# A fused attention and feed-forward kernel: two small loads on ScalarE's queue, one table zeroed by VectorE, and the first w3 tile ahead of w_out

## What is computed

```python
# attention, B=2, H=8, S=768, D=64, 16 centroids for each head
mask = argmax(q_n @ c_n) == argmax(k_n @ c_n)         # both normalised, as the centroids
attn = softmax(where(mask, q @ k.T / sqrt(D), -1e9))
x = (attn @ v)                                        # 1536 tokens x 512
# first feed-forward, d_ff=1024
h = ((x @ w1) * (x @ w2)) @ w3                        # w3: 1024 x 1024
y = h @ w_out                                         # w_out: 1024 x 512
# second feed-forward, d_ff=2048
g = x @ w_in; g = max(g, 0) + alpha * min(g, 0); out = g @ w_out2
```

## Time and profile before

| | us |
|---|---|
| median of three runs | 748.8 |
| the profiled execution | 748.81 |
| its span, first to last instruction | 747.0 |
| TensorE products busy (PE) | 740.9 (99%) |
| TensorE weight loads busy (PEld) | 641.8 (86%) |
| VectorE busy (DVE) | 414.1 (55%) |
| ScalarE busy (ACT) | 312.8 (42%) |
| GpSimd busy (POOL) | 179.7 (24%) |

### The profile page before, as it was taken

One profiled execution on the slowest core, in us unless ns is written; L12 is line 12 of the kernel. 1 busy time (PEld: TensorE's weight loads), 2 busy tenths in 40 slices (PEclk: granted clock), 3 DMA queues, 4 the chain that ended last, 5 costly groups with the idle time before them and its releaser, 6 DMA issues.

```text
span 747.0 us, 10658 instructions
## 1 busy us (share of the span) xinstructions
PE 740.9 (99%) x3792; PEld 641.8 (86%) x3792; DVE 414.1 (55%) x632; ACT 312.8 (42%) x623; POOL 179.7 (24%) x211
## 2 busy tenths in 40 slices
PE   8999999999999999999999999999999999999998
PEld 7888999999999998888888888888888888888886
DVE  4435999999999993721311432475433334343432
ACT  5235988988988884411311332432012111121111
POOL 2141466866865894500000000000000000000000
PEclk9999999999999999999999999999999999999999
DMA  9645476776576332300000032230001000010001
GB/s 296 193 127 126 84 164 135 146 163 150 130 165 152 73 87 84 106 29 1 1 0 1 13 100 70 72 117 25 1 0 57 1 0 1 1 56 1 1 0 57
DMA packets 64859, 55.74 MB, mean 75 GB/s; under 512 B 31520, under 2 KB 53040, under 8 KB 64816
## 3 DMA queue, kind: packets, MB, share of 16 engines
q1 hardware_dynamic: 64816, 55.16, 28.7%
HBM read 31.50 MB, written 3.19 MB: 46 GB/s over the span
## 4 chain that ended last, share of the span: by engine, by line
PE 97%; DVE 1%; POOL 1%; ACT 1%; issue 0%; POOLq 0%; DVEq 0%
PE slot L622 62%; PE acc L622 24%; PE slot L686 9%; PE acc L635 1%; PE slot L734 1%; DVE xl L1160 0%; DVE xl L1142 0%; POOL cwin L465 0%; ACT xh L935 0%; ACT xh L942 0%; POOL oh L466 0%; DVE abx L1280 0%; DVE ab L1276 0%; ACT abx L1052 0%; ACT asb L1038 0%
## 5 line engine op out<-in xcount | busy, mean ns | idle before, releaser
L622 PE MATMUL slot<-xh,w 128*128 128x512 f32 x768 | 247.9, 389 | 0.0
L622 PEld LDWEIGHTS slot<-xh,w 128*128 128x128 f32 x768 | 144.2, 188 | 29.8
L622 PE MATMUL slot<-xl,w 128*128 128x512 f32 x384 | 149.4, 389 | 0.0
L1098 ACT CAST gh<-gf 128x512 fp32r<-128x512 f32 x48 | 29.9, 623 | 203.2 <-PE acc L622 186.0
L1203 DVE TENSOR_TENSOR pl<-slot,ph 128x384 fp32r<-128x384 f32 x192 | 97.5, 549 | 8.4 <-ACT ph L970 8.2
L1197 DVE TENSOR_REDUCE nm<-slot 128x1 f32<-128x768 f32 x96 | 91.1, 949 | 15.3 <-PE slot L622 14.2
L970 ACT CAST ph<-slot 128x384 fp32r<-128x384 f32 x192 | 83.8, 489 | 33.3 <-PE slot L686 32.4
L962 ACT ACTIVATE pf<-slot,nm 128x768 f32<-128x768 f32 x96 | 88.2, 919 | 6.0 <-DVE nm L1197 5.7
L622 PEld LDWEIGHTS slot<-xl,w 128*128 128x128 f32 x384 | 72.1, 188 | 14.9
L1326 DVE TENSOR_TENSOR gl<-gf,gh 128x512 fp32r<-128x512 f32 x48 | 33.2, 692 | 89.9 <-ACT gh L1098 89.9
L622 PE MATMUL slot<-k,q 96*128 96x384 f32 (+1 forms) x384 | 83.0, 337 | 0.0
(11 more groups left out here) (121 smaller groups left out, 1015.9 us busy)
## 6 DMA issues: line engine op xcount, KB each, us to landing
stage<-in_moe_w SPq DMA_DIRECT2D x16, 256.0 KB, 3.2
stage<-in_moe_w_in SPq DMA_DIRECT2D x16, 256.0 KB, 2.7
stage<-in_moe_w_out SPq DMA_DIRECT2D x16, 256.0 KB, 3.0
stage<-in_moe_w SPq DMA_DIRECT2D x6, 512.0 KB, 4.2
qk<-in_q SPq DMA_DIRECT2D x16, 192.0 KB, 4.1
qk<-in_k SPq DMA_DIRECT2D x16, 192.0 KB, 4.3
vn<-in_v SPq DMA_DIRECT2D x16, 192.0 KB, 3.7
q<-k SPq DMA_DIRECT2D x16, 192.0 KB, 2.8
```

The source lines that it names most:

```text
L622: return nc.tensor.matmul(o, a, b, start=start, stop=stop)
L1098: copy(gh[j % 2][:, :], gf[j % 2][:, :]).then_inc(gh_done, 1)
```

## The change

The centroids' and alpha's loads are issued by ScalarE, ahead of its first wait, and no longer by SP. The zeros in `cwin[0]`, which the idle products read, are written by VectorE with a semaphore of their own, `zeroed`, and no longer by GpSimd, whose setup count falls by one. TensorE does 12 and 8 idle products in place of 8 and 6, and waits for the identity after the first group. ScalarE and VectorE take w3 tile 0 ahead of w_out piece 0. In `product_first` the pair with w3's low part comes before the pair with w_out's low part. Everything else is unchanged.

```diff
--- before.py
+++ after.py
@@ -205,7 +205,7 @@
         masked = [sem(f"masked{j}") for j in range(HB)]
         inverted, inverse_out, inverse_in = sem("inverted"), sem("inverse_out"), sem("inverse_in")
         low_in, join_in = ([sem(f"{name}{e}") for e in range(2)] for name in ("low_in", "join_in"))
-        setup_pool, setup_act = sem("setup_pool"), sem("setup_act")
+        setup_pool, setup_act, zeroed = sem("setup_pool"), sem("setup_act"), sem("zeroed")
         cen_turned, table_done = sem("cen_turned"), sem("table_done")
         piece_hi, piece_lo = sem("piece_hi"), sem("piece_lo")
         front_hi, front_lo = sem("front_hi"), sem("front_lo")
@@ -230,7 +230,7 @@
 
         block = ctx.enter_context(nc.Block())
 
-        POOL_SETUP = 16 + HB
+        POOL_SETUP = 15 + HB
         CEN_DVE = 6
         CLUS = 9
         W12_EARLY = len(W12_STEPS)
@@ -239,7 +239,7 @@
         NWO = NF // 2
         READY_W12, READY_W34 = NWO - W12_EARLY, NWO - W12_EARLY + NF
         W3_STAGED = 3
-        IDENT, ZEROS, OPERANDS = 2, 3, 5
+        IDENT, OPERANDS = 2, 4
 
         def staged(e, piece):
 
@@ -379,10 +379,8 @@
                 if c % T6 == 4 and (not last or c // T6 + 2 < HB):
                     next_v(it, c // T6 + 2)
 
-            sp.dma_start(cn[:, :], cen.rearrange("h c d -> (h c) d")).then_inc(ld_cen, 16)
             load_w3(0, 0)
             load_wo(0)
-            sp.dma_start(al16, alpha.rearrange("(j p) -> j p", p=P)).then_inc(ld_al, 16)
             for i in range(1, NWO):
                 load_wo(i)
             load_w3(1, 1)
@@ -454,7 +452,6 @@
             ordered(nc.gpsimd.memset(ident[:, :], 0.0))
             ordered(nc.gpsimd.affine_select(out=ident[:, :], in_=ident[:, :], compare_op=ALU.not_equal, fill=1.0,
                                             base=0, pattern=[[-1, P]], channel_multiplier=1))
-            ordered(nc.gpsimd.memset(cwin[0][:, :].bitcast(F32), 0.0))
             ordered(nc.gpsimd.memset(scl[:, :], 1.0))
             ordered(nc.gpsimd.memset(scl[0:D, :], SCALE))
             ordered(nc.gpsimd.memset(zero[:, :], 0.0))
@@ -751,12 +748,12 @@
                 pe.wait_ge(w3_hi, 1)
                 for g in range(2):
                     mm(o, w3h[:, 0, g, :], woh[:, g, :], g == 0, False)
+                pe.wait_ge(w3_lo, 1)
+                for g in range(2):
+                    mm(o, w3l[:, 0, g, :], woh[:, g, :], False, False)
                 pe.wait_ge(piece_lo, 1)
                 for g in range(2):
                     mm(o, w3h[:, 0, g, :], wol[:, g, :], False, False)
-                pe.wait_ge(w3_lo, 1)
-                for g in range(2):
-                    mm(o, w3l[:, 0, g, :], woh[:, g, :], False, False)
 
             def product_tile(f, parity):
                 pe.wait_ge(w3_lo, f + 1)
@@ -768,14 +765,15 @@
                 for _ in range(n):
                     mm(slot[2][:, 1, 0:HS], cwin[0][:, 0:P], cwin[0][:, 0:HS], True, True)
 
-            pe.wait_ge(setup_pool, ZEROS)
-            spin(8)
+            pe.wait_ge(zeroed, 1)
+            spin(12)
+            pe.wait_ge(setup_pool, IDENT)
             turn_w3(0, 0)
             pe.wait_ge(setup_act, 1)
             nc.tensor.transpose(acc[0:D, 0, 0:P], cn[:, :], ident[:, :])
             pe.wait_ge(ld_al, 16)
             nc.tensor.transpose(acc[:, 1, 0:NJ], al16, ident[0:NJ, 0:NJ]).then_inc(cen_turned, 1)
-            spin(6)
+            spin(8)
             product_first()
             pe.wait_ge(piece_lo, 2)
             product_wc(0, (2, 3))
@@ -922,6 +920,8 @@
         def _(act):
             copy = nc.scalar.copy
 
+            act.dma_start(cn[:, :], cen.rearrange("h c d -> (h c) d")).then_inc(ld_cen, 16)
+            act.dma_start(al16, alpha.rearrange("(j p) -> j p", p=P)).then_inc(ld_al, 16)
             act.wait_ge(ld_cen, 16)
             nc.scalar.activation(xf[0][:, 0, 0:D], cn[:, :], ACT.Square, accum_out=cs[:, 0:1]).then_inc(act_step, 1)
             act.wait_ge(dve_step, 1)
@@ -992,8 +992,8 @@
                     probabilities(it, c)
 
             act.wait_ge(setup_pool, OPERANDS)
+            w3_hi_part(0, 0)
             wo_hi(0)
-            w3_hi_part(0, 0)
             wo_hi(1)
             wo_hi(2)
             wo_hi(3)
@@ -1127,6 +1127,7 @@
                 dve.wait_ge(dve_step, count[0])
 
 
+            nc.vector.memset(f32(cwin[0][:, :]), 0.0).then_inc(zeroed, 1)
             dve.wait_ge(act_step, 1)
             ordered(nc.vector.tensor_scalar_max(cs[:, 1:2], cs[:, 0:1], 2.0 ** -100))
             dve.wait_ge(act_step, 2)
@@ -1226,8 +1227,8 @@
                     inverse(it, j)
 
             dve.wait_ge(setup_pool, OPERANDS)
+            w3_lo_part(0, 0)
             wo_lo(0)
-            w3_lo_part(0, 0)
             wo_lo(1)
             wo_lo(2)
             wo_lo(3)
```

## The result

The changed kernel takes 750.32 us (median of 15 runs, 750.12 to 750.50); the kernel before takes 748.80 in the same comparison. The ratio is 1.0019, with a 95% interval of 1.0013 to 1.0026: 1.5 us slower, a small loss that is clear of the measurement. The profiled execution took 750.23, its span is 748.4 (before: 748.81 and 747.0). The range given was 748.6 to 750.3, so the median lies 0.02 above its upper end, and it is 0.7 above the forecast of 749.6.

What follows compares the result with a forecast made beforehand. TensorE was taken to hold 97% of the chain, so only the start before 11.01 us could move; VectorE's first split 0.81 later gave 748.81 + 0.81 = 749.6 us, range 748.6 to 750.3.

Steps and rivals of the forecast that it cites:

- What bounds the kernel, and that the shift at 11.01 us carries over to the end: TensorE's products of chunk (2, 3) start at 11.01; the rest follows at the same distance, the later chain being TensorE.
- The loads, SP's side: SP's queue: w3 tile issued at 0.73 instead of 1.18, landing about 4.13; early[0] at about 5.8, later ones gain 0.9.
- The table load behind the issues: ScalarE's start: two issues until 1.63, table load of 1.28, Square at 2.92 in place of 2.48.
- The third rival: ScalarE: table load ahead of the two issues, up to +3.3, 752.1; with the second rival 0.14 to 750.3, 0.08 beyond.
- When the centroids land: Centroids on ScalarE's queue: landing bounded at 2.43 to 5.03; up to 3.8 was taken, costing nothing.
- The second rival: ScalarE's Square: centroids queue behind large transfers, landing L shifts L - 3.02; with the third 0.14 to 750.3, 0.08 beyond.
- The zeroed table: VectorE's memset begins at 0.73 and takes 0.35 to 0.42; TensorE's idle products start at about 1.18.
- Twelve idle products, and the clock: TensorE: twelve take 4.00, end at 5.18; transpositions take 1.91 at the lower clock, tile turned at 7.09.
- The first rival: TensorE's clock rises earlier, tile turned as early as 6.21: 748.5 to 749.3, chance 0.26.
- The order on ScalarE and VectorE: Turned w3 tile first: ScalarE starts it at 7.14, VectorE's first split at 8.27 against 7.46.
- the +0.81: Delay of VectorE's first split, moving TensorE's chunk (2, 3) products from 11.01 to 11.82.
- No effect on later work: After the first products everything else moves with the shift; transfers are earlier, so none becomes late.

Runs made afterwards that it cites:

- The run with the head start: Changed kernel with alpha's load as SP's first issue, ahead of w3 tile 0, centroids staying on ScalarE's queue: 749.33 us.
- the run with alpha moved: Kernel before with TensorE's order of w3 tile 0's products changed (high parts first) and alpha's load alone on ScalarE's queue: 747.57 us.

## Why the prediction was right and wrong, step by step

*What bounds the kernel, and that the shift at 11.01 us carries over to the end:* right. 1.58 at the first products, 1.59 at 18.85, 1.52 in the medians.

*The loads, SP's side:* right in the issues, wrong in the landing. The w3 tile and w_out's pieces were issued 0.45 and more earlier. But the w3 tile took 3.8 and not 3.4, since it shared the engines with the centroids: it landed at 4.53, where 4.13 was forecast and the kernel before has 4.58. Nothing hung on it, as TensorE's idle products ran on to 5.3.

*The table load behind the issues:* right, 1.66 to 2.94; the forecast had the Square possible at 2.92. The third rival is out.

*When the centroids land: the step that failed.* I bounded the landing at 2.43 to 5.03 and took "up to 3.8", so that it cost nothing, since the two issues start together. It was 4.70, and it decided the time. That they start together was the reason for the delay, not against it: the argument held only if a small transfer issued together with a large one were served ahead of it. The w3 tile's rows started first, and then the queues took turns row by row. The run with the head start shows it, 1.7 us to landing with the centroids issued by the same engine at the same moment; only alpha, behind them, had left their queue. The second rival had this place, this order of consequences and this price: L - 3.02 gives 1.68 for L = 4.70, measured 1.58 at TensorE's products. The 0.1 is that ScalarE starts the rounding at 7.92, while the scaling before it runs to 8.02; I had put them end to end. The rival had been given 0.14 (with the third, up to 750.3) and 0.08 (beyond), too little, and 750.32 lies on the border between the two.

*The zeroed table:* the memset took 0.38 (bounds 0.35 to 0.42), but began at 0.89 and not at 0.73, so the idle products began at 1.32 and not at 1.18.

*Twelve idle products, and the clock:* the start of the transpositions was forecast at 5.18 and was 5.33. That they take 1.91 was mis-sized: 1.42 in the changed kernel, so the tile was turned at 6.75 and not at 7.09. The first rival (an earlier rise of the clock) was there in this half measure. Against it I had set the distance of 6.2 us from the first product to the rise, taken from one execution. It did not carry over: in the changed kernel the last transpositions already ran at the 2.4 GHz pace by 6.75, 5.4 after its first product, and with the centroids back on SP all eight did, from 4.94 on, 3.6 after it. The early rise was hidden behind the centroids in the changed kernel. With them back on SP it fits the time of 748.91, where 749.2 to 749.6 was expected, but its profiled execution was a faster one (748.43).

*The order on ScalarE and VectorE:* the +0.81 was the sum of late idle products, low clock and order. In its place, the order alone measured +0.35 and the idle products alone 0.0, while with the centroids in time the two together, with alpha moved, gave +0.2; all three intervals take in no change. So +0.81 never appeared; the loss of 1.5 has another cause of about twice the size.

*No effect on later work:* right in the main; of the delay of 1.59 at 18.85, 0.2 had gone away by the end in the profiled pair.

The forecast, 749.6, therefore had the right sign and half of the size, by terms that did not appear. That the range all but reaches the measured time is luck as far as the forecast's own terms go: its upper end was there for the second rival, which I had made unlikely.

## What to carry to other kernels

A small transfer that something waits for should start ahead of the large ones, on whichever queue: the centroids took 1.7 us so, on SP's queue and on ScalarE's alike. Put on a second queue at the same moment as a large transfer, they started later and then went row for row with it, and landed 0.2 after it, at 4.70 against 4.53. What may land late is the safer thing to move: alpha alone on ScalarE's queue cost nothing that could be told. And where a product is split in parts of which one is late, give the in-order engine the others first: that was worth 1.1 us here.

## What the runs showed that I had not expected

Two queues on the same 16 engines shared by rows, not by bytes: 46 rows of 256 bytes for 46 of 4,096 in one half microsecond. Before that the second queue stood still: issued at the same moment, it moved nothing by 2.5 us while the other moved 31 rows (13 up to 2.0, then 18). Together, 32 KB took 4.0 us in place of 1.7.

The eight transpositions of w3 tile 0 took between 1.03 and 1.97 us in the profiles. In five of them TensorE had done the same eight idle products from 2.0 on and went straight on to the transpositions, and these took 1.91, 1.89, 1.76, 1.33 and 1.09: the clock's rise to the 2.4 GHz level falls at another place in each execution. It can also fall back. In the run with only the loads moved TensorE had nothing to do from 5.8 to 8.05, waiting for the centroids, and the products behind that gap run at the 1.2 GHz level again: the granted clock reads 0.54 from 8.05 to 10.6 and 0.50 from 10.6 to 11.4. In the changed kernel TensorE had nothing to do for 1.33 before the same place, and the products behind it kept the upper level (8 idle products in 1.69). TensorE's timeline of the run with only the loads moved (six idle products in 2.29, 1.33 in the run with alpha moved; two products of 512 columns in 1.05, later 0.63):

```profile
4.73 1.09 PE L732 MATMUL slot<-ident,stage 128*128 128x128 f32 x8
8.05 0.30 PE L773 MATMUL acc<-ident,cn 128*64 128x128 f32 x1 [2.23 <-ACT cn L930]
...
8.50 2.29 PE L620 MATMUL slot<-cwin 128*128 128x384 f32 x6
10.59 1.05 PE L620 MATMUL slot<-xh 128*128 128x512 f32 x2
...
12.02 0.63 PE L620 MATMUL slot<-xh,xl 128*128 128x512 f32 x2
```

In that run's chain TensorE works without a break from 8.57 on, so the lower level is on the path; yet the products of chunk (2, 3) start at 12.61, as late as the whole change's 12.59. Whether the lower level costs this run anything was not tested by itself.
